# Attention and two MLP layers on one core: the first layer's rows turned beside the scores, row copies moved up, the MLP begun a beat sooner, keys loaded at a beat's head

## The reference, cut to what matters

```python
# q, k, v: (4 batches, 8 heads, 576 rows, 64)
scores = q @ k.T / 8
scores = where(scores >= max(scores) - tau, scores, -1e9)
attn = softmax(scores)
x = (attn @ v) as (2304 tokens, 512)
h = x @ moe_w_in                       # 512 -> 2048
x = (s * relu(h)**2 + b) @ moe_w_out   # 2048 -> 512
h = x @ moe2_w_in
out = (h * sigmoid(1.702 * h)) @ moe2_w_out
```

## Time and profile before

| | |
|---|---|
| Median of 3 runs | 1076.37 us (1075.7 to 1076.7) |
| The profiled execution: its time | 1075.32 us |
| its span, first to last instruction | 1073.5 us |
| mean granted TensorE clock | 0.990 |
| PE matmul / PEld / DVE / ACT / POOL busy | 95% / 84% / 60% / 57% / 69% |

### The profile page before, as it was taken

The page is one execution under the profiler, slowest core; times in us unless marked ns, Lnnn a source line. Parts: engine busy times, 40 slices in busy tenths (PEclk is TensorE's granted clock), DMA queues, the critical chain, the costliest instruction groups (busy, mean ns, idle before and its releaser), DMA issues.

```text
span 1073.5 us, 17836 instructions
## 1 busy us (share of the span) xinstructions
PE 1023.5 (95%) x5824; PEld 906.7 (84%) x5824; DVE 643.4 (60%) x1480; ACT 610.9 (57%) x1151; POOL 744.5 (69%) x708
## 2 busy tenths in 40 slices
PE   5877999999998999999999999999999999999998
PEld 4656888878877888788889889899999999999997
DVE  7898999989988999899345454322222222222222
ACT  6765666656666666665455555545445454454543
POOL 5648887778777787776556566567666676666763
PEclk9988999999999999999999999999999999999999
DMA  5227877977886689768834344444444444454441
GB/s 195 64 65 183 233 202 199 232 214 184 235 200 157 182 225 224 194 169 203 184 113 134 118 122 121 116 135 149 127 129 150 135 148 131 125 151 134 147 133 55
DMA packets 107611, 169.42 MB, mean 158 GB/s; under 512 B 11392, under 2 KB 72960, under 8 KB 107520
## 3 DMA queue, kind: packets, MB, share of 16 engines
q1 hardware_dynamic: 107520, 168.28, 56.9%
HBM read 128.12 MB, written 4.72 MB: 124 GB/s over the span
## 4 chain that ended last, share of the span: by engine, by line
PE 79%; DVE 12%; SPq 3%; issue 3%; ACT 2%; DMA 1%; ACTq 0%; DVEq 0%
PE y_ps L609 33%; PE scores L590 24%; PE shared L590 9%; PE scores L501 5%; PE scores L556 4%; DVE scores L670 4%; DVE prob L694 3%; DVE blocks L708 3%; SPq L432 2%; PE shared L556 1%; DMA k_raw<-k 1%; PE shared L618 1%; DVE gate L725 1%; ACT rows_a L884 1%; DVE limit L677 1%
## 5 line engine op out<-in xcount | busy, mean ns | idle before, releaser
L988 POOL TENSOR_TENSOR w_lo<-w_raw,win_hi 128x512 fp32r<-128x512 f32 x192 | 277.4, 1445 | 94.8 <-ACT win_hi L845 89.0
L995 POOL TENSOR_TENSOR w_lo<-w_raw,wout_hi 128x512 fp32r<-128x512 f32 x192 | 247.2, 1287 | 95.9 <-ACT wout_hi L852 95.8
L728 DVE TENSOR_TENSOR gate<-scores,gate 128x384 f32<-128x384 f32 x96 | 53.5, 557 | 299.5 <-ACT gate L862 299.5
L609 PE MATMUL y_ps<-wout_hi,g_hi 128*128 128x512 f32 x576 | 227.9, 396 | 0.0
L609 PE MATMUL y_ps<-wout_hi,g_lo 128*128 128x512 f32 x576 | 227.5, 395 | 0.0
L609 PE MATMUL y_ps<-w_lo,g_hi 128*128 128x512 f32 x576 | 227.3, 395 | 0.0
L809 ACT ACTIVATE prob<-scores,neg_max 128x576 f32<-128x576 f32 (+1 forms) x160 | 118.8, 743 | 113.7 <-DVE scores L670 108.2
L590 PE MATMUL scores<-act_hi,w_lo 128*128 128x384 f32 x496 | 167.4, 337 | 0.0
L590 PE MATMUL scores<-act_hi,win_hi 128*128 128x384 f32 x496 | 167.1, 337 | 0.0
L590 PE MATMUL scores<-act_lo,win_hi 128*128 128x384 f32 x496 | 166.6, 336 | 0.0
L670 DVE TENSOR_SCALAR_CACHE_REDUCE scores<-scores,consts 128x576 f32<-128x576 f32 (+1 forms) x160 | 129.7, 811 | 24.2 <-PE scores L501 23.8
(11 more groups left out here) (69 smaller groups left out, 1750.8 us busy)
## 6 DMA issues: line engine op xcount, KB each, us to landing
w_raw<-slabs SPq DMA_DIRECT2D x190, 512.0 KB, 3.7
prob_t<-blocks SPq DMA_DIRECT2D x96, 120.0 KB, 3.1
k_raw<-k SPq DMA_DIRECT2D x32, 288.0 KB, 4.7
q_raw<-q SPq DMA_DIRECT2D x48, 192.0 KB, 4.1
prob_t<-blocks SPq DMA_DIRECT2D x96, 96.0 KB, 2.8
v_sb<-v SPq DMA_DIRECT2D x26, 320.0 KB, 5.1
prob_t<-blocks SPq DMA_DIRECT2D x96, 80.0 KB, 3.4
prob_t<-blocks SPq DMA_DIRECT2D x96, 64.0 KB, 3.2
```

The lines of the kernel that those rows point to most:

```text
L609: mm = nc.tensor.matmul(y_ps[g][:], gp[:, n % 2, toks], wp[:, :], start=(f == 0 and k == 0), stop=(f == SLABS - 1 and k == 2))
L988: nc.gpsimd.tensor_tensor(in_of(w_lo, n), in_of(w_raw, n), win_hi[n % IN_HI][:].bitcast(F32), ALU.subtract).then_inc(win_lo_ready, 1)
L995: nc.gpsimd.tensor_tensor(out_of(w_lo, n), out_of(w_raw, n), wout_hi[n % OUT_HI][:].bitcast(F32), ALU.subtract).then_inc(wout_lo_ready, 1)
```

## The change

1. `MLP_FROM` is 16: each step is one beat sooner and `FIRST_PURE` is 69. Tile ends while attention runs are now in beats 34, 50 and 66.
2. For the first-layer tiles 0 to 2 the turn rides ahead of the beat's first score tile. A beat turns two 128x128 blocks into columns 288 to 415 of the two banks of `scores[0]`, so a tile takes six beats (`RIDES`): 36 to 41, 52 to 57, 68 to 73. ACT and DVE take 128x2x128 each (`x_hi_riding`, `x_lo_riding`). DVE's mask of that tile waits for `x_hi`, and PE's next use of `scores[0]` waits for `x_lo`. h no longer waits for either.
3. The tiles 3 to 5 keep the old form with `shared`, in the steps 69 to 72, 85 to 88 and 101 to 104, two steps later behind the tile's end than before.
4. At a tile's end ACT copies the rows right behind `gated_hi`, then opens the gate; `slab_in_hi` goes to the next beat. In the steps behind attention the copy stays ahead of the gate and behind `slab_out_hi`.
5. SP loads a key at the head of its beat, ahead of the block moves, wherever the key's old slot is free by then.

```diff
-MLP_FROM = 17
+MLP_FROM = 16
+RIDES = GROUPS * DC // 2
 def turn_due(s):
     n = s - OUT_LAG
-    if n < SLABS:
+    done, f = n // SLABS - 1, n % SLABS
+    if not 0 <= done < LAYER_TILES:
         return None
-    done, f = n // SLABS - 1, n % SLABS
-    return (done, f) if done < LAYER_TILES and f < DC else None
+    if s - f + 1 + RIDES <= FIRST_PURE:
+        return (done, f - 1) if 1 <= f <= RIDES else None
+    return (done, f - 2) if s >= FIRST_PURE and 2 <= f < 2 + DC else None
...
             for beat in range(BEATS):
+                for e in range(2, HEADS):
+                    if max(0, key_split_beat(e) - 1) == beat and key_free_beat(e) <= beat:
+                        load_k(e)
                 for w in range(PE_GROUPS, len(GROUPS_OF)):
                     move_quads(w, beat)
...
                     pe.wait_ge(context_lo_ready, pieces_before(j // 2))
+                if j % 2 == 0 and turns_by(j // 2 - MLP_FROM - 1) > 0:
+                    pe.wait_ge(x_lo_ready, turns_by(j // 2 - MLP_FROM - 1))
...
+            def turn_riding(tile, r):
+
+                g, c = r // 2, r % 2 * 2
+                pe.wait_ge(y_copied, GROUPS * tile + g + 1)
+                for half in range(2):
+                    mm = nc.tensor.transpose(scores[0][:, half, HALF:HALF + P],
+                                             rows_a[:, g, (c + half) * P:(c + half + 1) * P], ident[:])
+                mm.then_inc(rows_turned, 1)
...
-            def turn_rows(tile, c, hidden_before):
+            def turn_rows(s, tile, c):
 
                 pe.wait_ge(y_copied, GROUPS * (tile + 1))
-                shared_free(min(hidden_before, FIRST_PURE), DC * tile + c)
+                pe.wait_ge(square_ready, FIRST_PURE)
+                pe.wait_ge(x_lo_ready, turns_by(s - 1))
...
+                if j % 2 == 0 and turn_due(j // 2 - MLP_FROM) is not None:
+                    dve.wait_ge(x_hi_ready, turns_by(j // 2 - MLP_FROM))
...
+                if tile_ends(s - 1) and s + 1 < STEPS:
+                    slab_in_hi(s + 1)
                 if s >= 1:
                     gated_hi(s - 1)
+                if tile_ends(s):
+                    copy_rows(s - OUT_LAG)
+                    if s < STEPS:
+                        gate_of(s)
                 if 0 <= s < STEPS:
                     slab_out_hi(s)
```

More of the change, by code:

```diff
@@ L133, in key_before, with key_free_beat @@
     return max((n for n in range(e) if key_slot(n) == key_slot(e)), default=None)
+def key_free_beat(e):
+    return key_tiles(key_before(e))[-1] // 2 + 1 if key_before(e) is not None else 0
 def key_split_beat(e):
@@ L248, in turn_due, with turns_for @@
     n = s - OUT_LAG
-    if n < SLABS:
-        return None
-    done, f = n // SLABS - 1, n % SLABS
-    return (done, f) if done < LAYER_TILES and f < DC else None
+    done, f = n // SLABS - 1, n % SLABS
+    if not 0 <= done < LAYER_TILES:
+        return None
+    if s - f + 1 + RIDES <= FIRST_PURE:
+        return (done, f - 1) if 1 <= f <= RIDES else None
+    return (done, f - 2) if s >= FIRST_PURE and 2 <= f < 2 + DC else None
 def turns_by(s):
     return sum(turn_due(n) is not None for n in range(s + 1))
+def turns_for(tile):
+    return sum(turn_due(n) is not None and turn_due(n)[0] <= tile for n in range(STEPS))
 def build(nc, q, k, v, consts_in, ident_in, slabs, out):
@@ L472, in _ @@
                 for e in range(2, HEADS):
-                    if max(0, key_split_beat(e) - 1) == beat:
+                    if key_split_beat(e) - 1 == beat and key_free_beat(e) > beat:
                         load_k(e)
@@ L631, in _ @@
             for beat in range(BEATS):
+                due = turn_due(beat - MLP_FROM)
                 for j in tiles_of(beat):
-                    if j < TILES or (j % 2 == 1 and riding(beat) is not None):
+                    if j < TILES or (j % 2 == 0 and due is not None) or (j % 2 == 1 and riding(beat) is not None):
                         buffer_free(j)
+                    if j % 2 == 0 and due is not None:
+                        turn_riding(*due)
                     if j % 2 == 1 and riding(beat) is not None:
@@ L644, in _ @@
             for s in range(FIRST_PURE, STEPS + OUT_LAG):
+                if turn_due(s) is not None:
+                    turn_rows(s, *turn_due(s))
                 mlp(s)
@@ L738, in gated_lo, with x_lo_riding, x_lo @@
                     nc.vector.tensor_tensor(g_lo[:, n % 2, :], g, hi, ALU.subtract).then_inc(g_lo_ready, 1)
-            def x_lo(tile, c):
-                dve.wait_ge(x_hi_ready, DC * tile + c + 1)
+            def x_lo_riding(s):
+                tile, r = turn_due(s)
+                c, start = r % 2 * 2, tile * TOK + r // 2 * P
+                dve.wait_ge(x_hi_ready, turns_by(s))
+                nc.vector.tensor_tensor(act_at(act_lo, slice(c, c + 2), start, P), scores[0][:, :, HALF:HALF + P],
+                                        act_at(act_hi, slice(c, c + 2), start, P).bitcast(F32),
+                                        ALU.subtract).then_inc(x_lo_ready, 1)
+            def x_lo(s):
+                tile, c = turn_due(s)
+                dve.wait_ge(x_hi_ready, turns_by(s))
                 nc.vector.tensor_tensor(act_at(act_lo, c, tile * TOK, TOK), shared[:, 0:TOK],
@@ L766, in _ @@
                         mask(j)
-                    if j % 2 == 0:
-                        rows_due(s)
+                    if j % 2 == 0 and turn_due(s) is not None:
+                        x_lo_riding(s)
                     if j % 2 == 0 and s >= 2:
@@ L778, in _ @@
                     gated(s - 1)
-                rows_due(s)
+                if turn_due(s) is not None:
+                    x_lo(s)
                 if s - 2 < STEPS:
@@ L922, in _ @@
                         copy_tail(j - 4)
-                    if j % 2 == 0:
-                        rows_due(s)
+                    if j % 2 == 0 and turn_due(s) is not None:
+                        x_hi_riding(s)
                 for j in tiles_of(beat, 4):
```

67 lines of the change are left out of this document (30 added, 37 removed).

## The result

The changed kernel takes 1066.21 us (median of 5 runs, 1062.29 to 1068.7), the kernel before 1075.7 in the same comparison: ratio 0.9907, 95% interval 0.988 to 0.9934, so 9.5 us faster where 19.9 were forecast. 1056 is missed, and so is the range (1051 to 1062). The profiled execution took 1063.62 us, its span is 1061.8, which is 11.7 less than before.

The account below looks back on a forecast made before the run. PE's own work was taken to set the pace in attention, and PE alone behind it. Turns -14.5, MLP start -3.7 and behind attention -1.7 make -19.9 from 1075.3: 1055.4, as a median 1056 us; range 1051 to 1062.

Parts of the forecast that it names:

- Keys at a beat's head: Key loads ahead of SP's block moves: frees 0.48 us of ACT, which is not the bound; no gain or cost taken.
- The prediction is wrong if the beats between the turns get longer: Failure sign in attention: longer beats there would say PE's standing had hidden work of DVE or of the DMAs.
- Turns of tiles 0 to 2: Turns during attention: 19.9 us of excess goes, 5.4 us of riding turns comes; net -14.5 us.
- The price of a turn: Each of 18 riding turns in attention was taken to cost 0.30 us, 5.4 us in all.
- over 6 as the sign of VectorE: Output starts in beats with a turn alone: 5.5 us apart expected; over 6 would mean VectorE binds.
- Row copies: ACT's tile-end copies behind `gated_hi`: a beat before the first turn, gate 1.5 us later at most; nothing by itself.
- MLP a beat sooner: MLP start: one 4.19 us step leaves the stretch behind attention; bounds -5.2 and -1.0, taken as -3.7 us.
- The stall in beat 32: First step of tile 1: PE would stand 1.5 us ahead of h, waiting for DVE's `act_lo`.
- Behind attention: Ends of tiles 4 and 5: 0.84 us of waiting for row copies goes at each; -1.7 us.
- VectorE's: Rival: VectorE bounds attention, so turns give back only its idle time; 1058.4, or 1059.5 us as a median; chance 0.2.
- The stall moved: Rival: stall moves to beat 32 and the late slab, start gains nothing; -12.4 us, 1064; chance 0.1.
- The slower rival: Rival: in 18 beats DVE's mask waits for ACT's `x_hi`; at 1.5 us each +7 us, 1083; chance 0.03.

Follow-up runs that it names:

- run 2: Changed kernel with all keys loaded at the beat's tail again, nothing else different: 1058.87 us, 18.4 us faster than the kernel before.
- run 6: Kernel before with only the keys loaded at the beat's head: 1079.84 us, 3.5 us slower than the kernel before.
- run 3: Changed kernel with the MLP beginning in beat 17 again, keys still at the head: 1065.43 us, 11.9 us faster than the kernel before.
- run 8: Changed kernel with keys at the tail and most later query and value data left out (wrong output): 1055.45 us, 20.9 us faster than the kernel before.
- run 12: Kernel before with most later query and value data left out (wrong output): 1076.87 us, ratio 1.0008 to the kernel before.
- run 1: Changed kernel measured again, unaltered, in a second comparison: 1064.59 us, 12.7 us faster than the kernel before.
- run 5: Kernel before with only the MLP beginning in beat 16: 1072.19 us, 4.2 us faster than the kernel before.
- run 7: Changed kernel with keys at the tail and the MLP from beat 17, so turns and row copies alone: 1061.65 us, 14.7 us faster than the kernel before.
- run 10: Changed kernel with keys at the tail and the slab loaded ahead of the block moves: 1058.55 us, 18.2 us faster than the kernel before.
- run 4: Changed kernel with most later query and value data left out, same number of DMA issues (wrong output): 1056.79 us, 20.5 us faster than the kernel before.
- run 13: Changed kernel with only the four keys of beats 50, 51, 65 and 66 at the tail: 1061.15 us, 15.7 us faster than the kernel before.
- run 14: Changed kernel with all keys at the tail except those of beats 50, 51, 65 and 66: 1061.77 us, 15.1 us faster than the kernel before.
- run 9: Changed kernel with keys loaded between block moves and slab from beat 16 on: 1060.28 us, 16.5 us faster than the kernel before.

## Why the prediction was wrong, point by point

- **Keys at a beat's head, "I take none": the step that failed.** It costs 5.7 us on the changed kernel (run 2) and 3.5 on the old (run 6). Without it the kernel takes 1058.9 us, inside the range, 18.4 faster where 19.9 were forecast. I asked only whether a key is *waited for* in SP's queue. What costs is what the key carries: 288 KB on DMA engines that the earlier trace rows show 0.74 to 0.80 busy on average and near full in the crowded beats. SP gives the key 0.38 us and goes on to the moves; their bytes come late. The Trainium skill (DMA: Bandwidth & Descriptors, section Queues, rings and completion order) says that each engine consumes a queue's descriptors in ring order. The traces fit in the window of 397 to 425 us: with the key ahead, 80 KB moves land after 5.2 us instead of 4.2 and slabs after 7.7 instead of 5.0. But run 3 has the keys ahead and slabs after 4.1, so one window is weak evidence; the waits summed over the whole trace (run 2) are stronger. The rows show lateness, not the rings themselves.
- **"The prediction is wrong if the beats between the turns get longer": they did**, by 0.78 and 2.84 us. The reason that I gave with it, that PE's stand had hidden work of the DMAs, holds in part at most: with the keys at the tail the 2.84 is 0.30 (and the 0.78 is 1.57), so most of the later one belongs to the key itself, and runs 8 and 12 leave some 2 us for what was hidden, not clear of their intervals. I had written this test down and put no price on it.
- **Turns of tiles 0 to 2, -14.5**: -12.7 in the changed kernel, -14.0 with the keys at the tail, by the table. (In the profile of run 1 it is -10.5.) The price of a turn was right: beats 36 to 41 take 40.80 us against 4 x 7.18 + 2 x 5.25 + 6 x 0.30 = 41.02. The turn alone takes 210.34 - 204.88 = 5.46 us where I said 5.5 and set over 6 as the sign of VectorE. The nine outputs at the lower clock are gone.
- **Row copies, nothing by itself**: 1.55 us behind `gated_hi`, not waited for in beat 52. Right as far as the timeline goes; it wasn't undone alone.
- **MLP a beat sooner, -3.7**: -4.2 alone (run 5), -3.7 between the medians of runs 7 and 2. By the output of beat 20 the profiled run is 108.59 - 107.45 = 1.14 us late, although a beat 8 that is 1.56 longer (5.82 us for 4.26), and no part of the change, stands ahead of it; so the start gained 0.4 of my 1 us. The profiles of runs 5 and 10 have a full clock in beat 8, and there the output of beat 20 stands 0.6 us ahead of that of before. The stall in beat 32 is 1.42 us in the timeline and 1.7 by the output starts, for 1.5.
- **Behind attention, -1.7**: the whole end gave -5.5 where -5.9 were forecast for it with the step; tile 4's step fell from 5.36 to 4.51, the 0.84 of the text. Right.
- **The rivals.** VectorE's (0.2) had the level of run 2 by accident, and its mark, over 6 us in beats with a turn alone, is not there (5.45 to 5.72 us in the changed profile). The Trainium skill (Perfetto Trace Analysis, section Identifying the Most-Contended Engine) names, beside the weight loads' share that the prediction quotes for this rival, a second measure for TensorE, the matmul FLOPs against the peak; no run here works it out. "The stall moved" (0.1) was nearest in time, 1064, and in part in kind: the late slab was in it; it doesn't name the moves. Its sum is wrong too: the -3.7 already holds the 1.5 us of beat 32, so only the lost gain of 1.0 and the 2 x 2.5 may be added, which gives -13.9 and 1062.5 as a median. That the printed 1064 lies nearer to the result is luck. The slower rival didn't occur: between 200 and 480 us no wait of DVE for `x_hi` is listed.
- **The sum by the runs**: -14.7 (run 7) - 3.7 + 5.7 = -12.7, the second comparison. These are differences of runs 7, 2 and 1 in a row, so the sum must come out; with run 5's -4.2 in place of the -3.7, measured by itself, it is -13.2. The first comparison gave -9.5; the changed kernel's ten times reach from 1061.5 to 1068.7, and what makes a run fall high or low within that was not settled.

Theory 1 stands in this form: bytes, not issues (run 4), and one shared shortage (runs 8 and 10). Open is how much of it was hidden before (runs 6 and 12), how the price spreads over the 26 keys (runs 13, 14), and which of slab and moves weighs more by itself (run 9).

## What to carry to other kernels

A load moved up a queue is not free because nobody waits for it; count the bytes that now stand ahead of every transfer behind it. When a stall of the pacing engine is removed, also ask which DMAs lived in its shadow: read the landing times and the DMA share of the beats around it, and redo them for a shorter beat. (These runs put a price of 5.7 us on the first; on the second they only hint.) Take an edit that "costs nothing" out of a bundle and run it alone: here that run would have shown the 3.5 us. Write the sign that would prove you wrong and then give it a number and a chance.

## What the hardware showed that I had not expected

The 16 DMA engines read as busy at very different rates. The busy digits and the rates of the 40 slices from 397 to 425 us, changed kernel:

```profile
DMA  0028987887959999999999999999999999999989
GB/s 0 0 56 171 194 167 155 180 181 164 149 222 402 323 324 303 318 235 178 131 212 197 201 296 202 214 220 294 238 140 220 191 263 257 226 252 244 231 190 286
```

Slices at digit 9 move from 131 to 402 GB/s; the low ones lie behind SP's issues of block moves. A mean rate of 211 GB/s looks like slack, and yet transfers came late here, with a busy share of 0.97; so the share is the row to read first. It is not a strict measure either: it counts the time that packets took and passes 1 in a crowded stretch (1.02 and 1.04 between 320 and 325 us). The second surprise is the clock between 40 and 45 us: 0.72 in the changed kernel's profile, that is 1.2 GHz for a part of it, and 1.00 in that of before, with PE busy 8.95 and 8.88 of the 10 us ahead of it. The lower clock cost 1.56 us (beat 8) and came with either start of the MLP; what decides it was not found.
